# Attention and two MLPs: the first segment's values and pooled outputs added by TensorE in PSUM, batch 1's tasks placed anew

## The reference

```
q_d, k_d, v_d = means of q, k, v over groups of 4 rows
out_up    = repeat(softmax(q_d k_d^T / 8) v_d, 4 times along the rows)
out_local = softmax(q k^T / 8 where |i - j| < 4) v        # a band of 7 offsets
x = out_up + out_local                    # as (2304, 512)
x = relu(x w_in)^2 w_out                  # 512 -> 2048 -> 512
out = max(x w1, x w2, x w3) w_out2        # 512 -> 768 -> 512
```

## Time and profile before

| what | value |
|---|---|
| median of 3 runs | 893.88 us |
| the profiled execution | 896.43 us, span 894.7 us |
| PE busy | 814.5 us (91%), 5438 matmuls |
| DVE busy | 501.0 us (56%) |
| ACT busy | 333.5 us (37%) |
| POOL busy | 230.0 us (26%) |
| chain that ended last | PE 76%, DVE 11%, ACT 3%, POOL 3% |

### The profile page before, as it was taken

One profiled execution on the slowest core, in us unless ns is written; L12 is line 12 of the kernel. 1 busy time (PEld: TensorE's weight loads), 2 busy tenths in 40 slices (PEclk: granted clock), 3 DMA queues, 4 the chain that ended last, 5 costly groups with the idle time before them and its releaser, 6 DMA issues.

```text
span 894.7 us, 13171 instructions
## 1 busy us (share of the span) xinstructions
PE 814.5 (91%) x5438; PEld 783.7 (88%) x5438; DVE 501.0 (56%) x514; ACT 333.5 (37%) x861; POOL 230.0 (26%) x199
## 2 busy tenths in 40 slices
PE   4625999989899999899999999899999999999994
PEld 4425999989788999888999999899999999999994
DVE  6998995797698949688859005812221212212220
ACT  3564255436454445455454543321111112121111
POOL 0878741335321236311236323200000000000000
PEclk9556999999999999999999999999999999999998
DMA  9910341011610014410010015311010201010001
GB/s 209 343 66 9 81 89 40 14 28 46 157 27 1 28 27 105 100 27 27 1 27 28 1 52 174 119 63 36 14 58 1 71 1 51 20 36 1 20 17 36
DMA packets 39984, 50.33 MB, mean 56 GB/s; under 512 B 9844, under 2 KB 30324, under 8 KB 39028
## 3 DMA queue, kind: packets, MB, share of 16 engines
q1 hardware_dynamic: 39764, 49.45, 20.0%
q10 hardware_dynamic: 160, 0.04, 0.0%
HBM read 37.98 MB, written 11.21 MB: 55 GB/s over the span
## 4 chain that ended last, share of the span: by engine, by line
PE 76%; DVE 11%; ACT 3%; POOL 3%; DMA 2%; SPq 2%; issue 1%; DVEq 0%; ACTq 0%
PE PS L453 24%; PE PS L455 23%; PE PS L454 23%; DVE tmp L866 3%; DVE qk L878 2%; DMA WOr<-moe_w_out 2%; PE PS L492 2%; PE PS L511 2%; ACT qkT L649 1%; POOL WI L1086 1%; PE PS L518 1%; PE PS L539 1%; PE PS L483 1%; POOL WO L1086 1%; PE PS L499 1%
## 5 line engine op out<-in xcount | busy, mean ns | idle before, releaser
L453 PE MATMUL PS<-XS,WI 128*128 128x288 f32 (+1 forms) x768 | 244.8, 319 | 2.9 <-DVE XS L1043 2.9
L454 PE MATMUL PS<-XS,WI 128*128 128x288 f32 (+1 forms) x768 | 240.7, 313 | 0.0
L455 PE MATMUL PS<-XS,WI 128*128 128x288 f32 (+1 forms) x768 | 240.6, 313 | 0.0
L1109 POOL TENSOR_TENSOR G<-g,G 128x288 fp32r<-128x288 f32 x128 | 146.7, 1147 | 279.7 <-ACT G L697 279.4
L453 PE MATMUL PS<-G,WO 128*128 128x288 f32 x512 | 159.0, 311 | 5.6 <-POOL G L1109 5.6
L454 PE MATMUL PS<-G,WO 128*128 128x288 f32 x512 | 153.6, 300 | 0.0
L455 PE MATMUL PS<-G,WO 128*128 128x288 f32 x512 | 153.2, 299 | 0.0
L453 PEld LDWEIGHTS PS<-XS,WI 128*128 128x128 f32 x768 | 146.8, 191 | 5.4 <-DVE XS L1043 3.1
L454 PEld LDWEIGHTS PS<-XS,WI 128*128 128x128 f32 x768 | 147.3, 192 | 1.5
L455 PEld LDWEIGHTS PS<-XS,WI 128*128 128x128 f32 x768 | 146.9, 191 | 0.0
L692 ACT ACTIVATE PS<-PS 128x288 f32<-128x288 f32 x128 | 50.8, 397 | 161.3 <-PE PS L455 150.3
(11 more groups left out here) (108 smaller groups left out, 1162.0 us busy)
## 6 DMA issues: line engine op xcount, KB each, us to landing
qk<-q SPq DMA_DIRECT2D x8, 576.0 KB, 5.2
vb<-v SPq DMA_DIRECT2D x4, 1152.0 KB, 7.8
x_scratch<-x2s SPq DMA_DIRECT2D x8, 576.0 KB, 3.5
XR<-x_scratch SPq DMA_DIRECT2D x6, 768.0 KB, 4.9
out<-osb SPq DMA_DIRECT2D x36, 128.0 KB
qk<-k SPq DMA_DIRECT2D x3, 1152.0 KB, 8.4
WIr<-moe_w_in SPq DMA_DIRECT2D x3, 1024.0 KB, 15.3
WOr<-moe_w_out SPq DMA_DIRECT2D x3, 1024.0 KB, 15.4
```

What stands on the lines that cost most here:

```text
L453: mm(dst, wt(HI), xt_(HI), start=first, stop=False)
L454: mm(dst, wt(HI), xt_(LO), start=False, stop=False)
L455: return mm(dst, wt(LO), xt_(HI), start=False, stop=last)
L1109: Q.tensor_tensor(G[:, s % NGR, LO], g32[:, s % 2], G[:, s % NGR, HI].bitcast(f32), ALU.subtract).then_inc(g_ready, 1)
```

## The change

Segment 0 alone: VectorE still makes the 7 products of probability and v, into four buffers in turn; TensorE adds them, by transposing each into the same PSUM banks without clearing (`add_weighted`: 9 transposes for each offset), so x comes out transposed and summed. The pooled outputs of batch 0 are added there too: ScalarE writes each head's scaled output twice (`od_two`), and TensorE multiplies it with a 0/1 matrix `spread` into the same banks (`add_pooled(h)` on TensorE: 3 matmuls for each head). The pooled query order of batch 0 is changed for this (80 partitions instead of 72). The reciprocals are taken for each head, straight from PSUM. The x of segment 0 is split into high and low parts straight from PSUM, by ScalarE and VectorE. q's rows of segment 0 are copied to PSUM by ScalarE, and VectorE reads them there from the second product on; the scores and statistics of segments 0 and 1 lie in PSUM.

`odg` for batch 0, which only segment 1 still needs, goes through DRAM: 8 stores and 8 loads instead of 16 moves. Its scaled copies lie where `g32` lies later, so the first square waits for the stores. v is loaded behind the first group of weights. 18 weight tiles are split ahead of the first step instead of 26, and then one a step instead of two. The tables move, too, and VectorE's order in batch 1.

```diff
-    QK_AT = {1: (1, 0, 0), 2: (2, 11, 0), 3: (4, 11, 0)}
-    HEADS_AT = {1: (1, 1, 3), 2: (2, 12, 2), 3: (4, 12, 2)}
+    QK_AT = {1: (1, 0, 1), 2: (2, 11, 0), 3: (4, 11, 0)}
+    HEADS_AT = {1: (1, 1, 3), 2: (2, 13, 0), 3: (4, 13, 0)}
-    X_AT = {0: [None, None, None, (0, 11, 3), (0, 12, 3), (0, 13, 3)],
-            1: [(1, 12, 3), (1, 13, 3), (1, 14, 3), (2, 4, 1), (2, 5, 1), (2, 6, 1)],
+    X_AT = {0: [None, None, None, (0, 15, 1), (0, 15, 2), (0, 15, 3)],
+            1: [(1, 13, 1), (1, 14, 0), (1, 14, 3), (2, 6, 1), (2, 7, 1), (2, 8, 1)],
-    EXP_AFTER = {1: 0, 2: 2, 3: 2}
-    EXP_AT = {(0, 2): 1, (1, 13): 3, (3, 13): 5, (5, 13): 7}
+    EXP_AFTER = {1: 4, 2: 2, 3: 2}
+    EXP_AT = {(0, 8): 1, (1, 15): 3, (3, 11): 5, (5, 11): 7}
-    W_AHEAD, W_BEFORE_X = 26, 22
+    W_AHEAD = 18
...
+            def add_weighted(o):                       # TensorE
+                pe.wait_ge(weighted_made, o + 1)
+                for x in X0:
...
+                    for m in range(m0, m1):
+                        last = mm(PS[:, ATT[bk], P * (m - m0):P * (m - m0 + 1)],
+                                  view(weighted(o)[:, 2 * m:2 * m + 2, :], "p r d -> p (r d)"), ident[:],
+                                  start=o == 0 and m == m0, stop=False, is_transpose=True)
+                last.then_inc(weighted_added, 1)
...
+            def add_pooled(h):                         # TensorE
+                read(pe, 0, ("o", h))
+                for x in X0:
...
+                    last = mm(dst, view(od_first(h, 0), "p r d -> p (r d)"), spread[:, m0:m1], start=False, stop=h == NH - 1)
...
+                    if b == 0:                         # ScalarE, task o
+                        act.wait_ge(head_normed, h + 1)
+                        for n in range(2):
+                            last = A(od_first(h, n), src, ACT.Copy, scale=hst[:, h, n:n + 1])
...
-            seg = value_steps(0, three)                # VectorE, segment 0
-            for h in range(3, NH):
-                run(seg, 2)
-                head_max(0, h)
-                if h >= 5 and h % 2:
-                    norm_pair((h - 5) // 2)
+            for o in range(BAND):
+                weight(o)
+                if o + 4 < NH:
+                    head_max(0, o + 4)
+                norm_head(o + 1)
...
-            run(seg, 5)
-            add_pooled(0)
-            evacuate_x(0, 1)
+            first_hi_part(0)
+            for t in (1, 2, 0):
+                first_lo_part(t)
+            dve.wait_ge(weighted_added, BAND)
...
                 if b in PE_SUMS:                       # VectorE, batch 1
                     run(seg, 9)
+                    head_max(b, 0)
                     pool_v(b)
+                    head_max(b, 1)
...
+                    run(seg, 4)
+                    scale_pooled(b)
...
+                if b in PE_SUMS:
+                    run(seg, 3)
+                    add_pooled(lo)
+                    run(seg)
+                    softmax_in(hi)
```

More of the change, by code:

```diff
@@ L68, in attention_and_two_mlps @@
     X0 = X[:len(X) // 2]
+    ADD_IN = {n: [("add", n - 4)] + [("pooled", n - 4)] for n in range(4, NH + 2)}
     heads0 = []
@@ L108, in attention_and_two_mlps @@
                 put(place, 0, b, X[t:t + 1])
-    SEQ = [(0, t) for t in first_tasks] + [bt for key in sorted(PLAN) for bt in PLAN[key]]
-    ATT = (6, 7, 0, 1, 2)
+    SEQ = [(0, t) for t in first_tasks if t[0] not in ("add", "pooled")] + [bt for key in sorted(PLAN) for bt in PLAN[key]]
+    ATT = (6, 7, 0, 1, 2, 4, 5)
     def bank_of(b, task):
@@ L380, in _ @@
                 load_w_out(n)
[L381 to L384, removed]
+                if n == 0:
+                    load_v(0)
+            two = view(od_two[:], "p (h n) r d -> p h n r d", n=2)
+            for h in range(NH - 2, -2, -2):
+                read(sp, 0, ("o", NH - 1 - h))
+                for n in range(2):
+                    part, cnt = q_part(0, n)
+                    skip = n * (2 * QB - SD)
+                    sp.dma_start(od_dram[0, h:h + 2, part.start + skip:part.stop, :].rearrange("h p d -> p h d"),
+                                 two[skip:, h:h + 2, n, 0]).then_inc(od0_stored, 16)
+            sp.wait_ge(od0_stored, 16 * NH)
+            for h in range(NH):
+                sp.dma_start(odg[h:P:NH], od_dram[0, NH - 1 - h].rearrange("(j g) d -> g j d", g=NG)).then_inc(od0_loaded, 16)
             for b in range(1, NB):
@@ L491, in attend @@
                     for n in range(2):
-                        last = mm(ps[:SB, n * SD:(n + 1) * SD], qkT[rows, 0, h // 2, n * SB:(n + 1) * SB],
+                        part, cnt = q_part(b, n)
+                        last = mm(ps[:cnt, n * SD:(n + 1) * SD], qkT[rows, 0, h // 2, part],
                                   qkT[rows, 1, h // 2, :], start=True, stop=True)
@@ L601, in _ @@
             pe.wait_ge(consts, 1)
-            for task in first_tasks:
-                attend(0, task)
+            for task in first_tasks[:-len(X0)]:
+                if task[0] == "add":
+                    add_weighted(task[1])
+                elif task[0] == "pooled":
+                    add_pooled(task[1])
+                else:
+                    attend(0, task)
             for s in range(TOTAL + LAG):
@@ L714, in copy_first @@
                 A(t32[:, s % 2], PS[:, UP2[(3 * s) % 4], :CT], ACT.Copy).then_inc(c_copied, 1)
-            def scale_pair(pair):
-                act.wait_ge(pair_normed, pair + 1)
-                rec = view(hst[:], "p h n -> p (h n)")
-                for c in range(4 * pair, 4 * pair + 4):
-                    last = A(od_st[:, c, :D], od_st[:, c, :D], ACT.Copy, scale=rec[:, c:c + 1])
-                last.then_inc(pair_scaled, 1)
             w = [0]
@@ L812, in product @@
                         dve.wait_ge(dve_step, made["sum", o - m])
-                    made["product", o] = count(V.tensor_tensor(own[o % m], qk[:, lo:hi, :],
+                    if n == 0 and o == 1:
+                        dve.wait_ge(q_copied, 1)
+                    made["product", o] = count(V.tensor_tensor(own[o % m], q_first if n == 0 and o else qk[:, lo:hi, :],
                                                                qk[:, K0 + lo + o:K0 + hi + o, :], ALU.mult))
@@ L1069, in _ @@
             Q.memset(mask[:], 0.0)
+            Q.memset(spread[:], 0.0)
             Q.memset(ident[:], 0.0).then_inc(made, 1)
@@ L1082, in _ @@
                             pattern=[[0, HALO], [0, BAND]], channel_multiplier=1).then_inc(consts, 1)
+            for r in range(2):
+                Q.affine_select(out=spread[:, r::2], in_=spread[:, r::2], compare_op=ALU.not_equal, fill=1.0, base=0,
+                                pattern=[[-NG, (HR // 2 + 1 - r) // 2], [-1, NG]], channel_multiplier=1).then_inc(spread_made, 1)
             def split_w(i):
```

251 lines of the change are left out of this document (149 added, 102 removed).

## The result

The changed kernel takes 909.4 us (median of 4 runs, 906.67 to 912.41) against 894.62 for the kernel before (4 runs, 891.91 to 895.4): a ratio of 1.0181 (95% interval 1.0157 to 1.0205). It is 1.8% slower, where 879 us were forecast, with a range of 864 to 893. The profiled execution is the fastest of the four, 906.67 us with a span of 904.6.

The account below looks back on a forecast made before the run. VectorE bounds segment 0; from 98 us TensorE is full except for waits. Of 24.1 us, 6.5 are given back and batch 1 leaves 3.9; with 4.8 and 6.2 that makes 14.9 gained: 881.5 profiled, 879 us median, range 864 to 893.

Parts of the forecast that it names:

- head cycle: TensorE's work per head in segment 0: 5.3 us at the low clock, about 3.0 at the full one.
- rival 1: Segment 0: the clock stays low throughout, head cycles take 5.3 us, everything 11 us later, total 890; chance 0.14.
- relu of step 6: The seventh MLP step's relu: at 79.4 us against 103.47, so 24.1 us early.
- scaling: Scaling of batch 1's pooled outputs on VectorE, when its ods are complete: 172.7 us instead of 190.28.
- scaling to segment 3's end: VectorE in batch 1: 55.0 us with 14 more steps of 1.3, ending segment 3 at 227.7 instead of 232.2.
- wait for pooled q and k: TensorE before batch 2's qk transposes: a new wait of 5.2 us, leaving 3.9 us gained.
- TensorE without gaps gets the full clock: Segment 0: gapless from about 34 us, TensorE's clock rises at 39, and the MLP starts at 58.2 instead of 75.19.
- Given back at the first chunk's end: TensorE waits 3.2 us there and loses 1.7 of clock besides a 1.6 wait: 6.5 of 24.1 us lost, 17.6 left.
- Batch 1's order: Scaling inside segment 2's values on VectorE eats most of the gain; 4.5 us are left in VectorE's time.
- Heads half a step later: Batches 2 and 3: TensorE's waits of 2.2 us shrink to 0.6, with the clock 2.4 each, 4.8 us gained.
- Exponential two steps earlier: Segment 5 ends 6.3 us earlier and TensorE's wait of 4.59 at 361.67 goes, with the clock 6.2 us gained.
- Rival 3: Segment 0: TensorE's queue and the VectorE/ScalarE loop add up, cycle 8.2 us, MLP at 89, total 910; chance 0.09.

Follow-up runs that it names:

- run 9: The changed kernel plus 80 dense matmuls, whose output nothing uses, in TensorE's waits between 21 and 34 us: 892.63 us, ratio 0.9997.
- run 10: run 7's kernel plus the same 80 dense matmuls as run 9: 869.75 us, ratio 0.9734.
- run 7: The changed kernel with VectorE's old batch 1 order and old or in-between table places, keeping segments 5 and 7's early exponentials: 887.2 us, ratio 0.9925.
- run 2: The changed kernel with VectorE's old batch 1 order and EXP_AFTER as before: 902.64 us, ratio 1.011 to the kernel before.
- run 14: run 9's kernel with VectorE's old batch 1 order (the edit of run 2), the change's tables kept: 882.48 us, ratio 0.9877.
- run 1: The kernel before with only VectorE's new batch 1 order and the EXP_AFTER 4 it needs: 909.4 us, ratio 1.0175.
- run 4: The kernel before with only the heads of batches 2 and 3 half a step later: 898.17 us, ratio 1.0051.
- run 3: The kernel before with only the exponentials of segments 5 and 7 two steps earlier: 887.62 us, ratio 0.9937.
- run 5: The changed kernel plus 36 dense matmuls in TensorE's waits between 21 and 33 us: one execution of 895.31 us, three of 909.84 to 912.56.
- run 6: run 5's kernel plus six short dense matmuls in each of three head cycles: four executions of 894.63 to 897.54 us, six of 908.35 to 912.66.
- run 8: run 7's kernel plus run 5's 36 dense matmuls: executions of 874.49, 875.01 and 886.14 us, and three of 889.03 to 889.98.
- run 12: run 10's kernel plus dense matmuls in two waits at the first up, and segment 3's exponential a step earlier: 865.14 us, ratio 0.9678.

## Why the prediction was wrong

What follows takes the prediction's steps in their order; run 9 is the case that the forecast supposed.

| step | predicted | the change | run 9, clock granted |
|---|---|---|---|
| first weighted product | 32.5 | 32.40 | 32.14 |
| head cycle | 3.0 (rival 1: 5.3) | 6.01 | 3.21 |
| relu of step 6 | 79.4 | 93.23 | 78.41 |
| first head_max of batch 1 | 132.0 | 149.38 | 134.52 |
| scaling | 172.7 | 190.28 | 176.84 |
| scaling to segment 3's end | 55.0 | 55.9 | 55.5 |
| wait for pooled q and k | 5.2 | 4.77 | 4.92 |
| total | 879 | 909.4 | 892.6 |

1. **The step that failed first is "TensorE without gaps gets the full clock ... I put the rise at 39 us".** TensorE had no gap from 34 us on, and its clock was 0.50 until 65.2. Run 9 shows that this cost 909.4 - 892.6 = 16.8 us (run 10 against run 7: some 17): more than rival 1's 11, since the cold cycle is 6.0 and not 5.3 (s 1.18, nine transposes 1.97, pooled 1.16, t 0.53, o 1.17 from start to start). What failed in the reasoning is the comparison: the `up` steps of the earlier trace rows are other matmuls. Which of the cycle's matmuls make the difference no run tests. Rival 1 had the mechanism, with a chance of 0.14. Against its own case the trace of before did hold a sign that I passed over: the clock falls ahead of the phase, in TensorE's waits (1.00 until 23 us), so the phase would begin at the low level:

```profile
23.00:24.00 1.00, 0.00 (x0) 0.00 (x0) 1.00 (x2) 0.00 (x0) 1.00 (x1) 0.81 1.04 240
24.00:34.00 10.00, 3.74 (x22) 3.02 (x23) 8.55 (x13) 2.92 (x8) 8.99 (x6) 0.50 1.05 322
```

The Trainium skill, "TensorE: Matmul & The Clock Gate", section "Why this matters for your kernels", advises to keep TensorE busy to get the full clock; by the change's own windows that isn't enough, as 18.00 of 18.00 us busy stood beside 0.50. The section "A second HAM failure mode: psum-queue depth-cycling" speaks of short idle times between groups; here the low clock lasted without any that the trace shows.

2. **Given back at the first chunk's end.** Predicted 6.5. In the change it was all 11.2, in run 9 from -26.4 to -13.4, so 13.0. I had the waits for `add_pooled` (2.2) and for the high part of x (3.65) in the sum, as 1.6 and 3.2, but not the one of 2.4 us for the copies of qkT: with `QK_AT` one place later, ScalarE's four copies to x2s (146.32) stand ahead of the last copy of qkT (147.50). Around this wait (steps 17 to 20) run 9's lead falls from 18.7 to 13.4. The lead ahead of it all was 26.4 where I had 24.1, so 4.2 us are what the 13.4 left miss of my 17.6.

3. **Batch 1's order.** The size was right: 55.0 predicted, 55.9 and 55.5 measured, 14 more than before. I called it the step that "eats most of the gain". What it costs at the end depends on the tables around it: 6.8 us in the change (run 2), 10.1 with the clock granted (run 14), 15.4 with the tables of before (run 1). The prediction never asked what it would cost on its own, which is what would have shown the change's downside.

4. **Heads half a step later.** Predicted 4.8 gained, measured 4.2 lost (run 4). I priced the waits that go and put 0.6 in their place (measured 0.67 and 0.65), without looking up who else waits at the new place: `o`, nine times, for ScalarE's copy of `t`. That turns the gain into a loss of some 2 us; the rest of the 4.2 is not explained.

5. **Exponential two steps earlier.** 6.2 predicted, 6.4 measured (run 3).

For run 9 the account closes: 4.2 (2) + 9.0 (4) is 13.2 of the 892.6 - 879 = 13.6 us. Here 9.0 is from run 4's median; in run 9's own ruler the heads cost 1.4 and 2.3 us where 4.8 were to be gained, which is 8.5. For the change the 16.8 of (1) come on top. Rival 3, the only one on the slower side, named 910 and missed its mechanism: TensorE's queue never stood still, and the cycle of 6.0 was work at half the clock.

Right were also: no stall of VectorE on the reciprocals (in the change 0.14 to 0.16 us each, but only the one at 36.10 met a split of GpSimd; in run 9 seven of eight pairs did, and took the same), one split a step on GpSimd, the MLP's start at a full clock (56.7 in run 9, 58.2 predicted).

Open: what decides at 30 us between runs 5 and 6, whose rows up to there are alike but for one wait (1.31 us before 24.85 in run 5, 1.98 before 24.44 in run 6), and what gave the clock back at 36 us in run 8 and at 65.2 in the change. With the waits filled all 28 executions came out in the fast group; no run shows how few matmuls would do, nor whether 36 do so on another chip.

## What to carry to other kernels

Where a phase shifts work to TensorE, price it at both clocks from the stretch ahead of it: what mattered here was the clock that it found, and the waits in front of it could be filled with matmuls that cost no time to be measured. Price every moved table entry and every changed order alone, with its sign when the gain it is meant to spend does not come. For each wait that goes, name the first instruction behind the new place, on all engines in whose queue something was moved, and what stands ahead of its operands there.

## What the hardware showed that was not expected

- TensorE busy for 34.94 of 35 us (run 6) at a granted clock of 0.50, and the same mix of work busy for 18.00 of 18 us at 1.00 (run 9). The level was kept in both stretches.
- With 36 dense matmuls in the waits one execution of four (run 5) and four of ten (run 6) were in the fast group, with 80 twelve of twelve (run 9). The time of one kernel had two values 14 us apart (run 8: 875.01 and 889.03), with mean granted clocks of 0.974 and 0.953; a trace is there only of a fast one.
- Two more dense bursts held the clock over waits of 2.65 and 0.87 us (run 10's trace) at the first `up`. Run 10's windows:

```profile
54.00:60.00 6.00, 2.92 (x11) 2.60 (x12) 5.72 (x16) 1.98 (x7) 2.00 (x2) 0.57 0.22 49
60.00:66.00 6.00, 6.00 (x30) 6.00 (x30) 6.00 (x5) 3.33 (x9) 3.25 (x4) 0.57 0.03 7
```

and run 12's:

```profile
54.00:60.00 6.00, 5.97 (x53) 5.10 (x51) 5.34 (x16) 3.04 (x9) 3.09 (x3) 1.00 0.20 45
60.00:66.00 6.00, 5.72 (x44) 5.61 (x43) 5.97 (x5) 4.68 (x12) 3.56 (x3) 1.00 0.10 22
```
